# Keeping the split weights of two expert passes in device memory, and moving one wait of TensorE from layer 1 to layer 2

## The chip, the cores and the metric

The program runs on one core of a Trainium2 chip. The metric is the device time of one execution in microseconds (us), the median over several runs. A core has the matrix engine TensorE (PE in the profile), the vector engine VectorE (DVE), ScalarE (ACT), GpSimd (POOL) and SyncE (SP), which here issues most of the transfers; 16 DMA engines carry them.

## The reference, cut to what matters

Three parts follow each other: a windowed attention with block summaries, a dense mixture of 4 experts, and a mixture of 8 experts in which each token goes to one. The change is in the dense mixture. It takes the 1536 rows of x (two batches of 768 rows, 512 wide) through every expert e:

```python
p = domain_probs / (domain_probs.sum(-1, keepdims=True) + 1e-09)
out = np.zeros((N, D), dtype=np.float32)
for e in range(E):                      # E = 4, D = 512, F = 1024
    h = np.maximum(x @ w1[e], 0.0)      # layer 1
    out += p[:, e:e + 1] * (h @ w2[e])  # layer 2
```

The weights of an expert are the same for both batches.

## The kernel before

**Three matmuls for one.** TensorE gets each float32 operand as a high part (rounded by ScalarE's copy) and a low part (the rest, a subtraction on VectorE); a product is hi·hi + hi·lo + lo·hi.

**Passes.** Expert 0, and expert 3 of the second batch, run in a plain form, in groups of 384 rows. The five others are passes, `PASSES` = (batch 0, experts 1, 2, 3), (batch 1, experts 1, 2), numbered t = 0 to 4; `SWITCH` = 3 is the first pass of batch 1. A pass does layer 1 for a whole batch with seven block products in the place of eight (a Strassen-Winograd scheme, so each w1 is needed as seven blocks A12, S1, A11, A22, S2, S4, S3: three are quarters of w1, four are sums or differences of quarters, 256x512 each; x as its quarters and four sums T1 to T4). It is done in four turns of seven products (`factors`, six matmuls each by two halves of the inner axis: 168 matmuls), and then layer 2 in six tiles of 128 rows (`rows_out`, 144 matmuls, 24 a tile).

**Layer 1's weights.** SP loads the four quarters of w1 into `w_raw` (`load_blocks`, semaphores `block_sent`) when all products of the pass before are through (`product`). VectorE makes four sums in place (`block_sums`), ScalarE copies each of the seven blocks to `wb_hi` (`high_block`), and VectorE subtracts (`low_blocks`), which puts `wb_lo` over `w_raw` and raises `block_ok`. All this lies in time beside layer 2 of the pass before: `between(t, tt)` says what VectorE does after it has added tile tt of pass t to `acc` (`add_more`, line 1370). TensorE may begin tile m when `rows_added` is m-1, since two PSUM banks take turns. `load_second` brings w2 of the pass into places of `acc` and `v2_raw_end` when layer 2 of the pass before is through (`rows_done`).

**The switch of batches.** At t = 3 the x of batch 1 comes back from `x_aside`, its four sums T1 to T4 are made again (`first_sum` and the like, line 1290 on, and their split `high_sum` and `low_sum`, line 1320), and the finished rows of batch 0 are stored.

**Order of work.** It is written out by hand for each engine. SP's list of transfers is one queue in order: a wait in it holds all that stands behind.

Of the kernel before, what the change touches and what calls it, by code (L numbers as in the profile page):

```python
# [7 lines left out]
F32 = mybir.dt.float32  # L8
# [7 lines left out]
P = 128  # L16


def sparse_attention_moe_moe(nc, q, k, v, dprobs, w1, w2, w_skip, w_gate, v1, v2, out):
# [28 lines left out]
    G = 4  # L48
    GT = N // G
    GR = GT // P  # L50
# [21 lines left out]
    HALF_F = F // 2  # L72
# [39 lines left out]
    x1_rows = nc.dram_tensor("x1_rows", (N, D), F32).ap()  # L112
    route_list = nc.dram_tensor("route_list", (QT * COLS, 2), F32).ap()
    x_aside = nc.dram_tensor("x_aside", (2, P, KC, S), F32).ap()

    qh = q.rearrange("b h s d -> (b h) s d")
    kh = k.rearrange("b h s d -> (b h) s d")
# [2 lines left out]
    with ExitStack() as ctx:  # L120
# [3 lines left out]
        def sem(name):  # L124
            return ctx.enter_context(nc.semaphore(name))
# [193 lines left out]
        def block_part(parts, k):  # L319
            return parts[:, k, :, :].rearrange("p c f -> p (c f)")  # L320

        def x_block(d, t):

            return tuple(x[:, HALF_D * d:HALF_D * (d + 1), t * GT:(t + 1) * GT].bitcast(F32) for x in (xt_hi, xt_lo))
# [54 lines left out]
            sem("l1_done"), sem("h_hi_ok"), sem("h_ok"), sem("l2_done"), sem("acc_ok"))  # L379
        x_saved, x_back, acc_saved, acc_back = sem("x_saved"), sem("x_back"), sem("acc_saved"), sem("acc_back")  # L380
        block_sent = [sem(f"block_sent{k}") for k in range(4)]
        block_sum, block_hi_ok, block_ok = sem("block_sum"), sem("block_hi_ok"), sem("block_ok")
        t_step, t_sum, t_pool, t_hi_ok, t_ok = sem("t_step"), sem("t_sum"), sem("t_pool"), sem("t_hi_ok"), sem("t_ok")
        product, put_by, joined = sem("product"), sem("put_by"), sem("joined")
        hb_hi_ok, hb_ok = sem("hb_hi_ok"), sem("hb_ok")
        v2_sent = [sem(f"v2_sent{k}") for k in range(3)]
# [30 lines left out]
        def _(sp):  # L417
# [108 lines left out]
            def load_blocks(t):  # L526

                w = w1[PASSES[t][1]]
                for k, (to, row, col) in enumerate(((A12, 1, 0), (S4, 0, 1), (A22, 1, 1), (A11, 0, 0))):
                    sp.dma_start(w_raw[:, to, :, :], w[row * HALF_D * P:(row + 1) * HALF_D * P, col * HALF_F:(col + 1) * HALF_F].rearrange(  # L530
                        "(c p) f -> p c f", p=P)).then_inc(block_sent[k], 16)

            def load_second(t):

                b, e = PASSES[t]
                at = v2_at(b, 0)
                for k in range(2):
                    sp.dma_start(acc[:, at + 3 * k:at + 3 * k + 3, :], w2[e][3 * k * P:(3 * k + 3) * P, :].rearrange("(f p) d -> p f d", p=P)).then_inc(v2_sent[k], 16)
                sp.dma_start(v2_raw_end[:, :, :], w2[e][6 * P:8 * P, :].rearrange("(f p) d -> p f d", p=P)).then_inc(v2_sent[2], 16)
# [48 lines left out]
            sp.dma_start(late, acc[:, TPH:2 * TPH, :]).then_inc(acc_saved, 16)  # L588
            sp.wait_ge(acc_saved, 16)
            load_second(0)  # L590
            for t in range(1, len(PASSES)):
                sp.wait_ge(product, BLOCKS * FP * t)
                load_blocks(t)
                if t == SWITCH:
                    for j, x in enumerate((xt_hi, xt_lo)):
                        sp.dma_start(x[:, 0:KC, :].bitcast(F32), x_aside[j]).then_inc(x_back, 16)
                sp.wait_ge(rows_done, TPH * t)
                if t == SWITCH:
                    sp.dma_start(acc[:, TPH:2 * TPH, :], late).then_inc(acc_back, 16)
                    for g in range(HALVES):  # L600
                        keep(g)
                        send_out(g)
                    sp.wait_ge(x1_kept, 16 * HALVES)
                    sp.wait_ge(x1_out, 16 * HALVES)
                    sp.wait_ge(x1_tr, TPH)
                load_second(t)
            sp.wait_ge(product, BLOCKS * FP * len(PASSES))
            for c in range(PIECES):
                sp.dma_start(stage[:, c, :], w1_piece(w1[E1 - 1], c)).then_inc(w1_in[c], 16)
# [196 lines left out]
        def _(act):  # L806
# [137 lines left out]
            def high_blocks(t):  # L944

                for j in BLOCK_ORDER:
                    high_block(t, j)
                    if t in (0, SWITCH) and j in T_AFTER:
                        high_sum(PASSES[t][0], T_AFTER[j])

# [59 lines left out]
            high_blocks(0)  # L1010
            for t in range(len(PASSES)):
                factors(t)
                if t + 1 < len(PASSES):
                    high_blocks(t + 1)
                if t >= SWITCH:
                    route_exp(t - SWITCH)
# [80 lines left out]
        def _(dve):  # L1097
# [239 lines left out]
            def low_blocks(t, part):  # L1337
                for k in part:
                    j = BLOCK_ORDER[k]
                    dve.wait_ge(block_hi_ok, BLOCKS * t + k + 1)  # L1340
                    TT(block_part(wb_lo, j), block_in(j), block_part(wb_hi, j).bitcast(F32), ALU.subtract).then_inc(block_ok, 1)  # L1341
                    if t in (0, SWITCH) and j in T_AFTER:
                        low_sum(PASSES[t][0], T_AFTER[j])

            def low_second(t, k):
                f = ROW_ORDER[k]
# [203 lines left out]

            def between(t, tt):

                if t + 1 == SWITCH:
                    if tt == 0:
                        block_sums(t + 1, 0)
                        block_sums(t + 1, 1)
                    if tt == 1:
                        low_blocks(t + 1, range(1))
                    if tt == 2:
                        first_sum(1)  # L1560
                        second_sum(1)
                    if tt == 3:
                        fourth_sum(1)
                        third_sum(1)
                    if tt == 4:
                        low_blocks(t + 1, range(1, 4))
                    if tt == 5:
                        low_blocks(t + 1, range(4, BLOCKS))
                    return
                if t + 1 < len(PASSES):  # L1570
                    if tt == 0:
                        block_sums(t + 1, 0)
                        block_sums(t + 1, 1)
                    if tt == 1:
                        low_blocks(t + 1, range(3))
                    if tt == 2 and t < SWITCH:
                        low_blocks(t + 1, range(3, BLOCKS))
                    if tt == 4 and t >= SWITCH:
                        low_blocks(t + 1, range(3, BLOCKS))
                elif tt == 1:  # L1580
                    low_w1(1, lambda j: stage[:, j, :], [0, 1, 2])
                if t >= SWITCH:
                    if tt == 0:
                        choose(t - SWITCH)
                    if tt == 2:
                        places(t - SWITCH)
                    if tt == 3:
                        enter(t - SWITCH)
                    if tt == 4:
                        early_sum(t - SWITCH)  # L1590
# [165 lines left out]
        def _(pe):  # L1756
# [256 lines left out]
            def block(t, j, i, moving, bank, onto=False):  # L2013

                hi, lo = moving
                if i == 0:
                    pe.wait_ge(block_ok, BLOCKS * t + BLOCK_ORDER.index(j) + 1)
# [40 lines left out]
            def rows_out(t, fill):  # L2058

                b = PASSES[t][0]  # L2060
                for tt in range(TPH):
                    m = TPH * t + tt
                    if m >= 2:
                        pe.wait_ge(rows_added, m - 1)
                    for k, f in enumerate(ROW_ORDER):
                        if tt == 0:
                            pe.wait_ge(v2_ok, FC * t + k + 1)
                        if tt == 0 and k % 2 == 0:
                            pe.wait_ge(hb_ok, 4 * FP * t + 2 * k + 4)
# [13 lines left out]
            pe.wait_ge(o_lo, TASKS)  # L2083
            pe.wait_ge(pt_ready, 2 * TASKS)
            pe.wait_ge(h_ok, 2 + FC * G)
            pe.wait_ge(acc_ok, 2 + GR * G)
            for t in range(len(PASSES)):
                factors(t, route_fill if t == SWITCH else lambda k: None)

# [174 lines left out]
```

## Time and profile before

| | |
|---|---|
| median of 3 runs | 738.4 us (737.93 to 740.21) |
| profiled execution | 737.88 us, its span 736.1 us, so 1.8 us lie around the span |
| TensorE busy | 707.5 us, 96% |
| VectorE, ScalarE, GpSimd busy | 427.6, 291.6, 68.1 us |
| moved by DMA | 101.60 MB, mean 138 GB/s |
| the five passes | from 216.4 to about 538 us of the span |

The busy shares are means over stages with different limits. How a stage moves the end is read from the waits of the engine that is busy nearly all the time.

### The profile page before, as it was taken

The page shows a single profiled execution, that of the slowest core. Times are in us where ns is not written, and L with a number is a line of the kernel's source. Part 1 is how long each engine was busy: PE and PEld are TensorE (multiplying, and loading weights), DVE is VectorE, ACT ScalarE, POOL GpSimd, SP SyncE. Part 2 cuts the span into 40 slices and gives each one's busy share as a digit, 9 for nine tenths or more (in the row PEclk, how much of TensorE's full clock was granted, in tenths as well). Part 3 has the DMA queues.
Part 4 walks back from the last instruction along what each step waited for, and adds up shares of the span by engine and source line. Part 5 has one row for each costly group of instructions (what it writes and reads, how often), then busy time and mean ns, then how long its engine had stood idle before and what let it go on. Part 6 is the DMA issues. An engine that isn't in the chain of part 4 may idle for free.

```text
span 736.1 us, 12384 instructions
## 1 busy us (share of the span) xinstructions
PE 707.5 (96%) x4530; PEld 583.7 (79%) x4531; DVE 427.6 (58%) x1061; ACT 291.6 (40%) x651; POOL 68.1 (9%) x97
## 2 busy tenths in 40 slices
PE   5789999999989999999999999999999999999997
PEld 4578898888979889989988897898898985444444
DVE  4877674452976764782769469666542255544341
ACT  3655454351436614632624455056031202533430
POOL 2612000000000000000000000200100012332221
PEclk9999999999999999999999999999999999999999
DMA  9894732111523303213070723123224279599900
GB/s 200 215 219 94 145 68 63 42 37 62 225 76 124 115 1 116 74 41 115 1 285 9 280 84 115 24 91 115 86 86 172 87 287 356 204 396 396 386 8 21
DMA packets 88240, 101.60 MB, mean 138 GB/s; under 512 B 54617, under 2 KB 54893, under 8 KB 87281
## 3 DMA queue, kind: packets, MB, share of 16 engines
q1 hardware_dynamic: 85520, 96.14, 40.5%
q0 software_dynamic: 2656, 4.66, 2.0%
q8 instruction: 35, 0.57, 0.3%
q14 instruction: 29, 0.23, 0.1%
HBM read 88.32 MB, written 12.96 MB: 138 GB/s over the span
## 4 chain that ended last, share of the span: by engine, by line
PE 78%; DVE 12%; DMA 5%; issue 2%; SPq 1%; ACT 1%; POOL 0%; POOLq 0%; DVEq 0%; ACTq 0%
PE ps L1761 14%; PE ps L1763 14%; PE ps L1762 14%; PE ps L2023 6%; PE ps L2025 6%; PE ps L2024 6%; PE ps L2172 4%; PE ps L2144 4%; DMA sets<-in_moe_w 3%; DVE wb_lo L1341 2%; PE ps L1823 1%; PE ps L1795 1%; PE ps L1969 1%; PE ps L1809 1%; DVE xt_lo L1320 1%
## 5 line engine op out<-in xcount | busy, mean ns | idle before, releaser
L2023 PE MATMUL ps<-xt_hi,wb_hi 128*128 128x384 f32 x280 | 94.1, 336 | 4.8 <-DVE acc L1206 3.0
L2025 PE MATMUL ps<-xt_hi,wb_lo 128*128 128x384 f32 x280 | 93.6, 334 | 0.0
L2024 PE MATMUL ps<-xt_lo,wb_hi 128*128 128x384 f32 x280 | 93.6, 334 | 0.0
L954 ACT ACTIVATE h_raw<-ps 128x384 f32<-128x384 f32 x80 | 39.3, 491 | 90.8 <-PE ps L2025 88.9
L1762 PE MATMUL ps<-v_lo_acc,hb_hi 128*128 128x512 f32 x180 | 70.1, 390 | 0.0
L1761 PE MATMUL ps<-xt_hi,w_hi 128*128 128x384 f32 x184 | 64.2, 349 | 0.3 <-DVE h_lo L1197 0.3
L1355 DVE TENSOR_TENSOR h_raw<-ps,h_raw 128x384 f32<-128x384 f32 x80 | 41.4, 553 | 37.3 <-PE ps L2025 37.3
L1763 PE MATMUL ps<-xt_hi,w_lo 128*128 128x384 f32 x184 | 61.8, 336 | 0.0
L890 ACT ACTIVATE h_hi<-ps 128x384 fp32r<-128x384 f32 x48 | 23.6, 492 | 96.2 <-PE ps L1763 71.0
L1762 PE MATMUL ps<-xt_lo,w_hi 128*128 128x384 f32 x184 | 61.6, 335 | 0.0
L960 ACT ACTIVATE hb_hi<-h_raw 128x384 fp32r<-128x384 f32 x80 | 40.9, 526 | 45.3 <-DVE h_raw L1355 45.2
L1761 PE MATMUL ps<-w_hi,h_hi 128*128 128x512 f32 x144 | 58.1, 404 | 0.0
L2023 PEld LDWEIGHTS ps<-xt_hi,wb_hi 128*128 128x128 f32 x280 | 52.6, 188 | 5.6 <-issue 3.4
L1763 PE MATMUL ps<-w_hi,h_lo 128*128 128x512 f32 x144 | 56.4, 391 | 0.0
L1762 PE MATMUL ps<-w_lo,h_hi 128*128 128x512 f32 x144 | 56.2, 390 | 0.0
L2024 PEld LDWEIGHTS ps<-xt_lo,wb_hi 128*128 128x128 f32 x280 | 52.6, 188 | 0.2
L2144 PE MATMUL ps<-sets,acc 128*64 128x512 f32 x224 | 51.6, 599 | 1.1 <-DVE sets L1702 0.6
L2025 PEld LDWEIGHTS ps<-xt_hi,wb_lo 128*128 128x128 f32 x280 | 52.6, 188 | 0.0
L2172 PE MATMUL ps<-sets,acc 128*64 128x256 f32 x448 | 51.6, 382 | 0.7 <-ACT acc L1041 0.7
L1370 DVE SCALAR_TENSOR_TENSOR acc<-ps,dp,acc 128x512 f32<-128x512 f32 x30 | 22.5, 750 | 48.1 <-PE ps L1763 48.1
L1360 DVE SCALAR_TENSOR_TENSOR hb_lo<-h_raw,hb_hi 128x384 fp32r<-128x384 f32 x80 | 42.2, 555 | 12.0 <-ACT hb_hi L960 11.9
L1197 DVE SCALAR_TENSOR_TENSOR h_lo<-ps,h_hi 128x384 fp32r<-128x384 f32 x48 | 26.6, 555 | 37.3 <-ACT h_hi L890 37.2
(268 smaller groups left out, 1402.9 us busy)
## 6 DMA issues: line engine op xcount, KB each, us to landing
sets<-in_moe_w SPq DMA_DIRECT2D x72, 512.0 KB, 5.0
w_raw<-in_moe_w SPq DMA_DIRECT2D x20, 512.0 KB, 5.3
acc<-in_moe_w SPq DMA_DIRECT2D x10, 768.0 KB, 5.3
stage<-in_moe_w SPq DMA_DIRECT2D x8, 512.0 KB, 4.5
stage<-in_k SPq DMA_DIRECT2D x16, 192.0 KB, 4.8
acc<-in_v SPq DMA_DIRECT2D x4, 768.0 KB, 6.8
x_rows<-acc SPq DMA_DIRECT2D x4, 768.0 KB, 6.7
out_rows<-acc SPq DMA_DIRECT2D x4, 768.0 KB, 8.3
```

Of the source, the lines that this page charges most:

```text
L954: nc.scalar.activation(h_raw[:, f, half * GT:(half + 1) * GT], ps[:, bank, 0:GT], ACT.Copy).then_inc(put_by, 1)
L960: nc.scalar.activation(hb_hi[cols], h_raw[cols], ACT.Relu).then_inc(hb_hi_ok, 1)
L1355: TT(to, ps[:, bank, 0:GT], to, ALU.add).then_inc(joined, 1)
L1360: nc.vector.scalar_tensor_tensor(out=hb_lo[cols], in0=h_raw[cols], scalar=0.0, in1=hb_hi[cols].bitcast(F32), op0=ALU.max, op1=ALU.subtract ...
L1761: mm(dst, a_hi, b_hi, start=start, stop=False)
L1762: mm(dst, a_hi, b_lo, start=False, stop=False)
L1763: return mm(dst, a_lo, b_hi, start=False, stop=stop)
L2023: mm(to, wb_hi[w], hi(c), start=(c == 0 and not onto), stop=False, skip_group_check=onto)
L2024: mm(to, wb_hi[w], lo(c), start=False, stop=False, skip_group_check=onto)
L2025: last = mm(to, wb_lo[w], hi(c), start=False, stop=(c == HALF_D - 1), skip_group_check=onto)
L2144: last = mm(ps[j * QT:(j + 1) * QT, 0, 0:FQ], xt2[:, from_c:from_c + QT], wset[:, 0, at:at + FQ], start=(c == 0), stop=(c == KC - 1))
L2172: last = mm(ps[j * QT:(j + 1) * QT, bank, 0:DQ], ht2[:, at:at + QT], wset[:, 0, to:to + DQ], start=(f == 0), stop=(f == FC - 1))
```

## The change

- After pass 0's and pass 1's split blocks are made, SP stores `wb_hi` and `wb_lo` to a new tensor `w_aside` in device memory (`save_blocks`): two DMAs a pass, each 128 x 7168 floats, 3.67 MB, one run of 28,672 bytes a partition. They stand behind `load_second` of the same pass.
- `load_blocks` of passes 1 and 2 waits, beside `product`, for these stores (`blocks_saved`).
- Passes 3 and 4 use experts 1 and 2 again. Their blocks come back by 14 DMAs of 0.52 MB each (`blocks_again`), straight to `wb_hi` and `wb_lo`; there is no `load_blocks`, no sum, no high and no low part of blocks for them. TensorE waits for the DMAs (`block_back`, three semaphores: A12; S1 and A11; the four others).
- At t = 3 the load of x stands ahead of the blocks' load, and VectorE's sums and low parts of x are spread anew over the tiles.
- TensorE's wait for the last additions of the plain groups (`acc_ok`) moves from ahead of pass 0's layer 1 to its layer 2.

```diff
@@ -530,6 +537,18 @@
+            def save_blocks(t):
+
+                sp.wait_ge(block_ok, BLOCKS * (t + 1))
+                for j, x in enumerate((wb_hi, wb_lo)):
+                    sp.dma_start(w_aside[t, j], x[:, :, :, :].bitcast(F32)).then_inc(blocks_saved, 16)
+
+            def blocks_again(t):
+
+                for j in BLOCK_ORDER:
+                    for k, x in enumerate((wb_hi, wb_lo)):
+                        sp.dma_start(x[:, j, :, :].bitcast(F32), w_aside[t - SWITCH, k, :, j]).then_inc(block_back[back_part(j)], 16)
@@ -588,12 +607,17 @@
             load_second(0)
+            save_blocks(0)
             for t in range(1, len(PASSES)):
                 sp.wait_ge(product, BLOCKS * FP * t)
-                load_blocks(t)
                 if t == SWITCH:
                     for j, x in enumerate((xt_hi, xt_lo)):
                         sp.dma_start(x[:, 0:KC, :].bitcast(F32), x_aside[j]).then_inc(x_back, 16)
+                if t >= SWITCH:
+                    blocks_again(t)
+                else:
+                    sp.wait_ge(blocks_saved, 32 * min(t, KEPT))
+                    load_blocks(t)
                 sp.wait_ge(rows_done, TPH * t)
...
                 load_second(t)
+                if t < KEPT:
+                    save_blocks(t)
@@ -1550,34 +1577,28 @@
             def between(t, tt):
 
-                if t + 1 == SWITCH:
-                    if tt == 0:
-                        block_sums(t + 1, 0)
-                        block_sums(t + 1, 1)
-                    if tt == 1:
-                        low_blocks(t + 1, range(1))
...
+                if t + 1 == SWITCH:
+                    if tt == 1:
+                        first_sum(1)
+                    if tt == 2:
+                        second_sum(1)
+                        fourth_sum(1)
+                        low_sum(1, T1)
+                    if tt == 3:
+                        third_sum(1)
+                        low_sum(1, T4)
+                    if tt == 4:
+                        low_sum(1, T2)
+                        low_sum(1, T3)
@@ -2058,6 +2082,8 @@
             def rows_out(t, fill):
 
                 b = PASSES[t][0]
+                if t == 0:
+                    pe.wait_ge(acc_ok, 2 + GR * G)
@@ -2083,7 +2109,6 @@
             pe.wait_ge(h_ok, 2 + FC * G)
-            pe.wait_ge(acc_ok, 2 + GR * G)
```

SP's queue from the end of the plain groups to the blocks of pass 1, before (w_raw is where the quarters of w1 land, v2_raw_end and the acc places where w2 lands):

```order
L588 DMA x1_rows<-acc 128x6x512 [waits acc_ok]
L538 DMA acc<-in_moe_w2 128x3x512 [waits acc_saved]
L538 DMA acc<-in_moe_w2 128x3x512
L539 DMA v2_raw_end<-in_moe_w2 128x2x512
L530 DMA w_raw<-in_moe_w1 128x2x512 [waits product]
L530 DMA w_raw<-in_moe_w1 128x2x512 x3
```

The same place in the changed kernel:

```order
L607 DMA x1_rows<-acc 128x6x512 [waits acc_ok]
L557 DMA acc<-in_moe_w2 128x3x512 [waits acc_saved]
L557 DMA acc<-in_moe_w2 128x3x512
L558 DMA v2_raw_end<-in_moe_w2 128x2x512
L544 DMA w_aside<-wb_hi 128x7168 [waits block_ok]
L544 DMA w_aside<-wb_lo 128x7168
L537 DMA w_raw<-in_moe_w1 128x2x512 [waits blocks_saved,product]
L537 DMA w_raw<-in_moe_w1 128x2x512 x3
```

Two large stores now stand between, and the load of w1's quarters waits for them as well as for the products.

VectorE at the switch, its last work beside layer 2 of pass 2 and the first of pass 3, before (wb_lo are low parts of blocks, xt_lo those of x's sums, acc is a tile's addition, h_raw a joining of layer 1):

```order
L1370 SCALAR_TENSOR_TENSOR acc<-ps,dp,acc 128x512 [waits rows_done]
L1341 TENSOR_TENSOR wb_lo<-w_raw,wb_hi 128x1024 [waits block_hi_ok]
L1320 TENSOR_TENSOR xt_lo<-x_raw,xt_hi 128x768 [waits t_hi_ok]
L1341 TENSOR_TENSOR wb_lo<-w_raw,wb_hi 128x1024 [waits block_hi_ok] x2
L1320 TENSOR_TENSOR xt_lo<-x_raw,xt_hi 128x768 [waits t_hi_ok]
L1355 TENSOR_TENSOR h_raw<-ps,h_raw 128x384 [waits put_by,product]
```

The same place in the changed kernel:

```order
L1397 SCALAR_TENSOR_TENSOR acc<-ps,dp,acc 128x512 [waits rows_done]
L1347 TENSOR_TENSOR xt_lo<-x_raw,xt_hi 128x768 [waits t_hi_ok] x2
L1397 SCALAR_TENSOR_TENSOR acc<-ps,dp,acc 128x512 [waits rows_done]
L1382 TENSOR_TENSOR h_raw<-ps,h_raw 128x384 [waits put_by,product]
L1387 SCALAR_TENSOR_TENSOR hb_lo<-h_raw,hb_hi 128x384 [waits hb_hi_ok]
```

Nothing stands any more between the last tile's addition and the first joining of pass 3.

## Rows read from the trace of the kernel before

**Rows 1.** The page, busy time of the engines

```profile
PE 707.5 (96%) x4530; PEld 583.7 (79%) x4531; DVE 427.6 (58%) x1061; ACT 291.6 (40%) x651; POOL 68.1 (9%) x97
```

**Rows 2.** Windows: layer 1 of pass 0, and of pass 3 (stretch, length, busy times, clock, DMA)

```profile
213.60:245.80 32.20, 29.36 (x169) 29.39 (x170) 20.44 (x39) 16.87 (x35) 0.00 (x0) 1.00 0.32 115
402.40:443.00 40.60, 38.86 (x248) 38.21 (x248) 24.05 (x41) 20.11 (x42) 0.00 (x0) 1.00 0.50 170
```

**Rows 3.** Timeline before pass 0: start, length, engine, line, idle before and releaser

```profile
215.44 0.74 DVE L1206 TENSOR_SCALAR acc<-ps,dp 128x512 f32<-128x512 f32 x1
216.44 0.41 PE L2023 MATMUL ps<-xt_hi,wb_hi 128*128 128x384 f32 x1 [3.02 <-DVE acc L1206]
```

**Rows 4.** Timeline at the start of pass 3, VectorE and TensorE

```profile
405.43 2.36 DVE L1341 TENSOR_TENSOR wb_lo<-w_raw,wb_hi 128x1024 fp32r<-128x1024 f32 x2
408.57 0.56 DVE L1355 TENSOR_TENSOR h_raw<-ps,h_raw 128x384 f32<-128x384 f32 x1
...
407.11 0.34 PE L2025 MATMUL ps<-xt_hi,wb_lo 128*128 128x384 f32 x1
409.18 0.45 PE L2023 MATMUL ps<-xt_hi,wb_hi 128*128 128x384 f32 x1 [1.74 <-DVE h_raw L1355]
```

**Rows 5.** Instructions on tile w_raw: ns min/median/max of one

```profile
L935 ACT ACTIVATE wb_hi<-w_raw x35: 1041/1046/1064, 197.5 to 454.6; 128x1024 fp32r<-128x1024 f32 x35
L1341 DVE TENSOR_TENSOR wb_lo<-w_raw,wb_hi x35: 1214/1219/1225, 202.7 to 473.8; 128x1024 fp32r<-128x1024 f32 x35
```

**Rows 6.** ScalarE's first high part of w2 in pass 0; landing of DMAs on acc, 216 to 240

```profile
226.50 0.64 ACT L968 ACTIVATE v_hi_first<-acc 128x512 fp32r<-128x512 f32 x1
...
DMA to landing us min/median/max: 4.5/5.8/7.2
```

**Rows 7.** Timeline of SP's DMA issues

```profile
179.61 1.93 SPq L530 DMA_DIRECT2D w_raw<-in_moe_w  x4
...
222.00 1.37 SPq L538 DMA_DIRECT2D acc<-in_moe_w  x2
223.42 0.49 SPq L539 DMA_DIRECT2D v_raw_end<-in_moe_w  x1
245.83 1.91 SPq L530 DMA_DIRECT2D w_raw<-in_moe_w  x4
...
278.59 0.90 SPq L538 DMA_DIRECT2D acc<-in_moe_w  x2
...
307.74 1.91 SPq L530 DMA_DIRECT2D w_raw<-in_moe_w  x4
...
369.65 1.90 SPq L530 DMA_DIRECT2D w_raw<-in_moe_w  x4
```

**Rows 8.** Stores of x aside: issue time; size and us to landing; then w2's last part

```profile
L544 SPq DMA_DIRECT2D x_aside<-xt_lo x1: 438/438/438, 182.1 to 182.1; - x1
...
x_aside<-xt_lo SPq DMA_DIRECT2D x1, 1536.0 KB, 15.1
...
v_raw_end<-in_moe_w SPq DMA_DIRECT2D x1, 512.0 KB, 7.5
```

**Rows 9.** Windows: DMA rate (last number, GB/s) in stores of x and of acc

```profile
190.00:192.00 2.00, 2.00 (x13) 2.00 (x12) 1.68 (x4) 0.49 (x1) 0.00 (x0) 1.00 0.95 406
192.00:194.00 2.00, 2.00 (x14) 2.00 (x13) 1.97 (x3) 0.49 (x1) 0.00 (x0) 1.00 1.06 444
218.00:220.00 2.00, 2.00 (x14) 2.00 (x13) 0.10 (x1) 0.74 (x2) 0.00 (x0) 1.00 1.02 378
```

**Rows 10.** Timeline beside layer 2 of pass 0: first block sum, second addition, fourth tile

```profile
253.02 1.22 DVE L1327 TENSOR_TENSOR w_raw<-w_raw 128x1024 f32<-128x1024 f32 x1 [0.93 <-DMA w_raw<-in_moe_w]
257.92 0.74 DVE L1370 SCALAR_TENSOR_TENSOR acc<-ps,dp,acc 128x512 f32<-128x512 f32 x1
...
262.04 0.39 PE L1761 MATMUL ps<-v_hi_first,hb_hi 128*128 128x512 f32 x1
```

**Rows 11.** Window in the routed stage: DMA rate of loads of 4 KB runs

```profile
650.00:660.00 10.00, 10.00 (x74) 5.13 (x72) 4.80 (x11) 4.15 (x5) 4.19 (x4) 1.00 1.04 394
```

More of the change, by code:

```diff
@@ L114, in sparse_attention_moe_moe @@
     x_aside = nc.dram_tensor("x_aside", (2, P, KC, S), F32).ap()
+    KEPT = len(PASSES) - SWITCH
+    w_aside = nc.dram_tensor("w_aside", (KEPT, 2, P, BLOCKS, HALF_D, HALF_F), F32).ap()
     qh = q.rearrange("b h s d -> (b h) s d")
@@ L320, in block_part, with back_part @@
             return parts[:, k, :, :].rearrange("p c f -> p (c f)")
+        def back_part(j):
+            return 0 if j == A12 else 1 if j in (S1, A11) else 2
         def x_block(d, t):
@@ L381, in sparse_attention_moe_moe @@
         block_sent = [sem(f"block_sent{k}") for k in range(4)]
+        blocks_saved = sem("blocks_saved")
+        block_back = [sem(f"block_back{k}") for k in range(3)]
         block_sum, block_hi_ok, block_ok = sem("block_sum"), sem("block_hi_ok"), sem("block_ok")
-        t_step, t_sum, t_pool, t_hi_ok, t_ok = sem("t_step"), sem("t_sum"), sem("t_pool"), sem("t_hi_ok"), sem("t_ok")
+        t_step, t_sum, t_hi_ok, t_ok = sem("t_step"), sem("t_sum"), sem("t_hi_ok"), sem("t_ok")
         product, put_by, joined = sem("product"), sem("put_by"), sem("joined")
@@ L946, in high_blocks @@
                 for j in BLOCK_ORDER:
-                    high_block(t, j)
+                    if t < SWITCH:
+                        high_block(t, j)
                     if t in (0, SWITCH) and j in T_AFTER:
@@ L1012, in _ @@
                 factors(t)
-                if t + 1 < len(PASSES):
+                if t + 1 <= SWITCH:
                     high_blocks(t + 1)
@@ L1341, in low_blocks @@
                     TT(block_part(wb_lo, j), block_in(j), block_part(wb_hi, j).bitcast(F32), ALU.subtract).then_inc(block_ok, 1)
-                    if t in (0, SWITCH) and j in T_AFTER:
-                        low_sum(PASSES[t][0], T_AFTER[j])
+                    if t == 0 and j in T_AFTER:
+                        low_sum(0, T_AFTER[j])
             def low_second(t, k):
@@ L1551, in between @@
             def between(t, tt):
-                if t + 1 == SWITCH:
-                    if tt == 0:
-                        block_sums(t + 1, 0)
-                        block_sums(t + 1, 1)
-                    if tt == 1:
-                        low_blocks(t + 1, range(1))
[L1559 to L1570, printed above, removed]
+                if t + 1 < SWITCH:
                     if tt == 0:
@@ L1575, in between @@
                         low_blocks(t + 1, range(3))
-                    if tt == 2 and t < SWITCH:
+                    if tt == 2:
                         low_blocks(t + 1, range(3, BLOCKS))
-                    if tt == 4 and t >= SWITCH:
-                        low_blocks(t + 1, range(3, BLOCKS))
-                elif tt == 1:
+                if t + 1 == SWITCH:
+                    if tt == 1:
+                        first_sum(1)
+                    if tt == 2:
+                        second_sum(1)
[7 more added lines that the diff above has]
+                        low_sum(1, T3)
+                if t + 1 == len(PASSES) and tt == 1:
                     low_w1(1, lambda j: stage[:, j, :], [0, 1, 2])
@@ L2016, in block @@
                 if i == 0:
-                    pe.wait_ge(block_ok, BLOCKS * t + BLOCK_ORDER.index(j) + 1)
+                    if t < SWITCH:
+                        pe.wait_ge(block_ok, BLOCKS * t + BLOCK_ORDER.index(j) + 1)
+                    else:
+                        pe.wait_ge(block_back[back_part(j)], 32 * (1, 2, 4)[back_part(j)] * (t - SWITCH + 1))
                     if t in (0, SWITCH) and j in T_AFTER:
```

## The prediction

> **What bounds the kernel now.** The page first: TensorE is busy 96% of the span, VectorE and ScalarE 58% and 40% [rows 1]. So what these two are spared is worth nothing by itself; only the gaps of TensorE count, and I looked for them with the windows, one for each half of a pass, and the waits of PE in each. In all five passes TensorE loses about 5 us, at two places that the change touches. In the window of pass 0's layer 1 it is busy 29.36 of 32.20 us, in that of pass 3's layer 1 38.86 of 40.60 [rows 2]. The others are full, but for 0.3 us at the first tile of pass 3's layer 2.
>
> The first gap is 3.02 us: pass 0's first product waits for VectorE's last plain addition, which ends at 216.1, behind block work [rows 3]. The second is 1.74 us: TensorE's fifth product of pass 3 waits for the joining that stands on VectorE behind four low parts of blocks and x's sums; these end at 408.57, where the joining begins [rows 4]. Both show VectorE late at a boundary. What follows has to be read from SP's queue, since that is where the change puts its new work.
>
> **Part 1, block work left out in passes 3 and 4.** VectorE is spared 2 x (4 sums + 7 low parts) at 1.22 us, 26.8 us, and ScalarE 2 x 7 x 1.05 = 14.7 us [rows 5]. Beside layer 2 of pass 3 they hid behind full TensorE: nothing. At the switch the 1.74 us go: in the new order nothing stands between the last addition and the joining, and x's sums are spread over the four tiles before. Nothing else of that boundary is near: ScalarE waited on VectorE there too. I take -1.7 us.
>
> **Part 2, the blocks' way back.** At the switch 3.15 MB of x and 7.34 MB of blocks (14 x 0.52) are loaded, issued from 369.65 [rows 7] by 16 issues of some 0.48 us. At 394 GB/s, the rate of loads in 4 KB runs [rows 11], 10.5 MB take 26.6 us; with 5.4 us for start and end (worked out below) all have landed at 401.7. Pass 3 begins at 402.3, the fourth product, the first that wants the last group, some 4 us later. The cover is thin for the last blocks (4 to 5 us) and wide for A12. Before pass 4 there are 7.34 MB, 24 us in a stretch of 33: hidden. If the rate fell to 330 GB/s, 5.2 us would be added at the switch and the cover would just be gone. Cost taken: 0.
>
> **Part 3, TensorE's wait moved.** Pass 0's layer 1 can start 3.0 us earlier; its blocks are ready (the last low part and the sum T4's are wanted six products later). But SP's order is unchanged: w2's first part is issued at 222.00 and lands 4.5 us later, at 226.5, the moment when ScalarE starts its high part [rows 6, 7]. Moved 3 us ahead, ScalarE stands in this wait, and behind it in its list are the high part of the hidden rows and the `put` copies that free TensorE's banks; w2's second part (landing 7.2 us after 222.4 [rows 6]) is met the same way at 229.6. Following that chain, VectorE's joinings come at 230.7 where they were at 230.9. So TensorE keeps about 0.8 us of the 3.0 (from 0.5 up to all of it, if ScalarE's order gives more slack than I see).
>
> **Part 4, the stores.** Pass 0's two stores, 7.34 MB, stand behind w2's three loads (2.10 MB, issued from 222.00, last landing 223.42 + 7.5 = 230.9 [rows 7, 8]) and ahead of w1's quarters for pass 1, which were issued at 245.83 when layer 1 was through. When do they land? The nearest rows are x's stores: runs of 12 KB a partition, 406 to 444 GB/s [rows 9], I take 428. From 179.61, the first issue, to the last landing at 182.1 + 15.1 = 197.2 [rows 7, 8] a load of 2.10 MB and stores of 3.15 MB take 17.6 us; 5.24 MB at 428 are 12.2, so start, change from loads to stores, and last landing cost 5.4. Here: 9.44 MB / 428 = 22.1, + 5.4, from 222.0: 249.5. Worked from the other end: stores flow from some 229.5, 17.1 us, + 1.5 for the change + 2.2 for the last landing: 250.3. I take 250.0, with 247.5 (no loss but the landing) and 253.0 (378 GB/s, acc's store in 2 KB runs [rows 9]) as bounds.
>
> So w1's quarters are issued 4.2 us later than before. Who waits: VectorE's sums stand in its list between the first and the second tile's additions, and start when the quarters land, at 253.02; the second addition ends at 257.92 + 0.7, 12.8 us behind the issue (a later pass shows 12.2), and TensorE begins the fourth tile at 262.04, which needs that addition [rows 7, 10]. The issue may come at 262.0 - 12.5 = 249.5 and cost nothing against before; with 250.0 TensorE is 0.5 us behind the old kernel there, whatever it had gained at the start. The gain of part 3 is thus eaten by the store: **+0.5 us** for parts 3 and 4 together, from -0.8 to +3.5.
>
> Pass 1's stores: w2 is issued at 278.59, layer 1 ends at 307.74 [rows 7], so 29.1 us and the same 3.7 us of slack; 9.44 MB want 27.5 to 29. Hidden, and still so at 378 GB/s (31).
>
> **What the skill says of the rate.** The Trainium skill, "DMA: Bandwidth & Descriptors", Specifications, gives about 358 GB/s as HBM's limit for a core; its page "HBM Reference" (Specifications) limits this to both cores of a pair at work and has about 425 for one alone. The trace agrees with the second: 406 to 444. By the first the stores would take 20.5 us in place of 17.1, which would add 3.4 us.
>
> **Sum.** -1.74 + 0.5 = -1.2 us (part 2 adds 0). Against the profiled execution's own time, 737.88: **736.7 us**. This execution is 0.5 us below the median shown (738.4); a median of the new kernel may lie as much above my figure. What comes behind pass 4 is tied to TensorE's steps and moves with it.
>
> **Rivals.**
> - *Both gaps are given back.* If the stores land by 248, the issue costs nothing and part 3's gain stays: -1.7 - 0.8 to -1.7 - 1.5, so 734.7 to 735.4. If ScalarE had slack too and the stores landed by 246.3, all 4.8 us: 733.1. For it: runs of 28 KB, the longest in the program, may go faster than those of 12. Against: 7.34 MB in 17 us is already the best rate seen.
> - *The stores are slow* (the other side). Loads and stores mixed run slower in this trace, and no store of this length is in it. One mechanism: the store of pass 0 holds w1's quarters, VectorE stands in the wait for them, the second addition is late, and TensorE stops at the fourth tile of layer 2. Each us of landing beyond 249.5 is one us; it outweighs the 1.7 from a landing at 251.2, and gives over 2.2 us from 253.4, which is 375 GB/s by the same sum. At 330 GB/s: landing 255.1, +5.6 - 1.7, and pass 1 adds 0.5: 742. At 230 GB/s: 14.8 us more in pass 0, 10 in pass 1, 762.
> - *The stores run a sixth slower than x's*, at some steady ceiling: 17.1 us become 20.5, the landing 253.4, +3.9 - 1.7 = +2.2, 740.1. For it, acc's stores at 378 GB/s [rows 9]; against it, x's at 406 to 444. This is what the Trainium skill's first limit above would do.
> - *The blocks come back late at pass 3*, TensorE waiting on `block_back`: below 330 GB/s only. It would come along with slow stores.
>
> **How the numbers follow.** About 0.3%, 2.2 us, is what a measurement of this kernel tells from no change. Forecast, landing from 249 to 253, net -2.2 to +2.0: 0.52. Gaps given back: 0.26, of which all of it 0.04. Stores slow: 0.14. A sixth slower: 0.08, half of it over +2.2. Faster then is 0.28, same 0.53, slower 0.19. The range goes from 734.6 (the first rival's near end) to 741.5 (stores near 335 GB/s); about 0.1 lies beyond each end.
>
> **What would show it.** Pass 0's first product at about 213.4, without the wait for `acc`. ScalarE's first high part of w2 still at 226.5, now after a wait for a DMA. Two stores with a last landing near 250, and w1's quarters issued then, not at the end of layer 1. VectorE waiting some 4 us for `w_raw` beside layer 2 of pass 0, and TensorE a new wait of about 1.3 us (0.8 + 0.5) on `acc` at its fourth tile. No such wait in pass 1. No wait at pass 3's fifth product, and none on blocks. I am wrong if stores run below 375 or above 450 GB/s, if TensorE keeps more of the first 3 us, or if transfers of this size slow the engines' own instructions.

## The result, and the profile of the changed kernel

The changed kernel takes 737.5 us (median of 20 runs, 735.54 to 739.88), the kernel before 739.41 in 20 runs beside it (736.84 to 742.14). The ratio of the runs taken side by side is 0.997, 95% interval 0.9958 to 0.9983: 2.2 us less, from 1.3 to 3.1 (the two medians are 1.9 apart). The profiled execution took 737.65 us, its span 735.9.

The page first: span, busy times, one group of layer 2 and the DMAs of the change (KB each, us to landing).

```profile
span 735.9 us, 12370 instructions
...
PE 708.9 (96%) x4530; PEld 585.1 (80%) x4531; DVE 402.9 (55%) x1039; ACT 277.6 (38%) x637; POOL 66.3 (9%) x97
...
L1782 PE MATMUL ps<-v_hi_first,hb_hi 128*128 128x512 f32 x120 | 47.2, 393 | 1.5 <-DVE acc L1397 1.5
...
w_aside<-wb_hi SPq DMA_DIRECT2D x2, 3584.0 KB, 16.6
w_aside<-wb_lo SPq DMA_DIRECT2D x2, 3584.0 KB, 24.8
wb_hi<-w_aside SPq DMA_DIRECT2D x14, 512.0 KB, 11.9
```

Against [rows 1] VectorE has 22 instructions and 24.7 us less, ScalarE 14 and 14.0 us less. TensorE has as many matmuls as before, and a wait of 1.5 us at layer 2 that it did not have.

The waits of TensorE from the start of pass 0 to the start of pass 1's first sums (213 to 265 us): for what, us in total, times, longest.

```profile
PE ps L1782 <- DVE acc L1397: 1.5, 1, 1.5
PE ps L2047 <- ACT h_raw L981: 1.4, 1, 1.4
PE ps L2047 <- DVE h_raw L1382: 0.4, 1, 0.4
```

In place of one wait of 3.02 us [rows 3] there are three, 3.2 us together (ps is the bank in PSUM that a matmul writes, h_raw the joined sums of layer 1). The timeline shows where they stand: the last plain matmul, the first product right behind it, two products at layer 1, and the fourth tile of layer 2.

```profile
213.99 0.39 PE L1784 MATMUL ps<-w_hi,h_lo 128*128 128x512 f32 x1
214.22 0.33 PE L2047 MATMUL ps<-xt_hi,wb_hi 128*128 128x384 f32 x1
...
229.30 0.45 PE L2047 MATMUL ps<-xt_hi,wb_hi 128*128 128x384 f32 x1 [1.37 <-ACT h_raw L981]
...
232.02 0.45 PE L2047 MATMUL ps<-xt_hi,wb_hi 128*128 128x384 f32 x1 [0.35 <-DVE h_raw L1382]
...
263.72 0.50 PE L1782 MATMUL ps<-v_hi_first,hb_hi 128*128 128x512 f32 x1 [1.50 <-DVE acc L1397]
```

ScalarE and VectorE show what is late behind each. ScalarE stands 3.16 us in the wait for w2's first part, and once more for its second, with the copies that free TensorE's banks behind it; VectorE waits 5.90 us for w1's quarters, and the second addition starts at 262.92.

```profile
227.45 0.63 ACT L995 ACTIVATE v_hi_first<-acc 128x512 fp32r<-128x512 f32 x1 [3.16 <-DMA acc<-in_moe_w]
...
230.14 0.63 ACT L995 ACTIVATE v_hi_next<-acc 128x512 fp32r<-128x512 f32 x1 [0.90 <-DMA acc<-in_moe_w]
...
258.00 1.23 DVE L1354 TENSOR_TENSOR w_raw<-w_raw 128x1024 f32<-128x1024 f32 x1 [5.90 <-DMA w_raw<-in_moe_w]
...
262.92 0.75 DVE L1397 SCALAR_TENSOR_TENSOR acc<-ps,dp,acc 128x512 f32<-128x512 f32 x1
```

SP's issues give the landings: w1's quarters go out as soon as the last store has landed, 24.7 us behind its issue at 225.33 (the page's 24.8 is the median of pass 0's and pass 1's).

```profile
222.97 0.92 SPq L557 DMA_DIRECT2D acc<-in_moe_w  x2
223.93 0.49 SPq L558 DMA_DIRECT2D v_raw_end<-in_moe_w  x1
224.46 0.82 SPq L544 DMA_DIRECT2D w_aside<-wb_hi  x1
225.33 0.46 SPq L544 DMA_DIRECT2D w_aside<-wb_lo  x1
250.15 1.92 SPq L537 DMA_DIRECT2D w_raw<-in_moe_w  x4
...
280.38 0.90 SPq L557 DMA_DIRECT2D acc<-in_moe_w  x2
```

Windows over the stores, over the end of the blocks' way back, and over layer 1 of pass 3 (the last two numbers are the DMA share and GB/s, the one before them the clock):

```profile
235.00:237.00 2.00, 2.00 (x14) 2.00 (x13) 1.16 (x2) 1.45 (x4) 0.00 (x0) 1.00 1.06 459
...
243.00:245.00 2.00, 2.00 (x14) 2.00 (x13) 1.19 (x3) 1.24 (x3) 0.00 (x0) 1.00 0.94 401
...
396.00:398.00 2.00, 2.00 (x10) 1.65 (x10) 1.77 (x2) 0.85 (x1) 0.00 (x0) 1.00 1.04 416
398.00:400.00 2.00, 2.00 (x11) 1.64 (x10) 1.25 (x2) 0.00 (x0) 0.00 (x0) 1.00 0.31 125
...
404.19:441.31 37.12, 37.12 (x241) 37.08 (x241) 17.18 (x32) 19.44 (x40) 0.00 (x0) 1.00 0.52 185
```

The last block's issue stands at 383.88 and its landing 16.8 us behind, at 400.7, 3.5 us before pass 3, and in its layer 1 TensorE is full: the 1.74 us of [rows 4] are gone.

**Two stretches to compare by.** The whole times of two kernels differ by little more than their scatter, and in the profiles below pass 0 begins anywhere from 212 to 216 us, whatever the kernel; that is settled before 180 us, where the kernels are alike (section on the hardware). So I compare two stretches. **A** runs from the start of TensorE's last plain matmul to SP's issue of w2 for pass 1, that is over the seam and all of pass 0. **B** runs from the end of pass 2 (SP's `acc<-x_rows`) to the end of pass 3's layer 1 (SP's next issue for weights). By the single profile of before, A went from 65.56 (213.03 to 278.59) to 66.39 (213.99 to 280.38), +0.8; B from 39.12 (402.41 to 441.53) to 37.12, -2.0. Together -1.2, what was forecast, where the timed runs say -2.2. Between A and B, and from B to the end, the two are equal within 0.1 us; up to A's start the changed profile is 0.96 longer, which is the scatter just named. That the one profile gives just what was forecast is in part luck; the runs below show why the timed runs say more.

### The profile page after: what moved, and what is told of

Its sections match the earlier page's. It is cut to its first block, busy times and chain, and to the rows that moved or that the text cites. A ratio compares the mean times of both kernels' runs of the same rounds, so it can differ in the third digit from the quotient of the medians.

```text
span 735.9 us, 12370 instructions
## 1 busy us (share of the span) xinstructions
PE 708.9 (96%) x4530; PEld 585.1 (80%) x4531; DVE 402.9 (55%) x1039; ACT 277.6 (38%) x637; POOL 66.3 (9%) x97
## 4 chain that ended last, share of the span: by engine, by line
PE 76%; DVE 10%; DMA 9%; issue 2%; SPq 1%; ACT 1%; POOL 0%; DVEq 0%; POOLq 0%
PE ps L1782 14%; PE ps L1784 14%; PE ps L1783 14%; PE ps L2047 5%; PE ps L2049 5%; PE ps L2048 5%; PE ps L2197 4%; PE ps L2169 4%; DMA w_aside<-wb_lo 3%; DMA sets<-in_moe_w 3%; PE ps L1844 2%; PE ps L1816 2%; PE ps L1990 1%; PE ps L1830 1%; DVE wb_lo L1368 1%
## 5 line engine op out<-in xcount | busy, mean ns | idle before, releaser
L1782 PE MATMUL ps<-xt_hi,w_hi 128*128 128x384 f32 x184 | 64.2, 349 | 0.3 <-DVE h_lo L1224 0.3
L1782 PE MATMUL ps<-v_hi_first,hb_hi 128*128 128x512 f32 x120 | 47.2, 393 | 1.5 <-DVE acc L1397 1.5
## 6 DMA issues: line engine op xcount, KB each, us to landing
w_aside<-wb_lo SPq DMA_DIRECT2D x2, 3584.0 KB, 24.8
```

The lines of the kernel that those rows point to most:

```text
L1782: mm(dst, a_hi, b_hi, start=start, stop=False)
```

## The experiments

All of them, with what the profile of each gave. "Clock" is the granted TensorE clock between 217 and 223 us. The ratio of each run is to executions of the kernel before taken beside it, whose medians were 739.41 for the changed kernel, 739.93 for no_store0, wait_back, wait_only and store_twice, 739.98 for low_first, low_first_early, after_again and wait_back_again, and 740.35 for the last four. So two runs of different groups are compared by their ratios, not by their medians.

| kernel | median us | ratio to before (interval) | A | B | clock |
|---|---|---|---|---|---|
| before | 739.41 | 1 | 65.56 | 39.12 | 1.00 |
| changed | 737.5 | 0.997 (0.9958 to 0.9983) | 66.39 | 37.12 | 1.00 |
| no_store0 | (718.9) | not comparable | 64.34 | 37.11 | 1.00 |
| wait_back | 738.17 | 0.9983 (0.9968 to 0.9998) | 67.15 | 37.11 | 0.72 |
| wait_only | 737.6 | 0.9976 (0.9951 to 1.0001) | 64.37 | 39.12 | 1.00 |
| store_twice | 754.56 | 1.0202 (1.0179 to 1.0224) | 84.73 | 37.11 | 1.00 |
| low_first | 735.6 | 0.9937 (0.9914 to 0.9959) | 65.18 | 37.11 | 1.00 |
| low_first_early | 734.16 | 0.9906 (0.9875 to 0.9937) | 62.87 | 37.11 | 1.00 |
| after_again | 737.64 | 0.9966 (0.9944 to 0.9989) | 65.78 | 37.11 | 1.00 |
| wait_back_again | 738.55 | 0.9965 (0.9946 to 0.9985) | 68.23 | 37.12 | 0.52 |
| before_again | 739.63 | 0.9995 (0.9965 to 1.0024) | 66.92 | 39.12 | 0.78 |
| before_again_2 | 739.8 | 0.9992 (0.9964 to 1.002) | 67.12 | 39.12 | 0.72 |
| busy_switch | 738.53 | 0.9972 (0.9951 to 0.9993) | 65.35 | 38.35 | 1.00 |
| best_again | 733.38 | 0.9906 (0.9875 to 0.9937) | 62.82 | 37.11 | 1.00 |

**1. No store in pass 0** (no_store0). The changed kernel without pass 0's two stores. Pass 3 then takes the blocks of expert 2 in the place of expert 1's, so the routed stage sorts its tokens otherwise and takes another time: the whole time can't be compared, A can.

```diff
             load_second(0)
-            save_blocks(0)
...
-                if t < KEPT:
+                if t == 1:
                     save_blocks(t)
```

> The changed kernel without pass 0's stores; passes 3 and 4 both take pass 1's blocks, so pass 3 computes with another expert's w1 and the loads stay as many. Yardstick, in each profile: from TensorE's last plain matmul to the issue of pass 1's w2 (before 65.6 us, changed 66.4). Theory (the store holds w1's quarters, and that alone makes the wait at the fourth tile): quarters issued at the end of layer 1, no wait at the fourth tile, yardstick 64.7; the switch as in the changed kernel; whole time 1.7 us under the changed kernel's, some 2.9 us or 0.4% under before. Rival (pass 0 is late for w2's landing alone): the yardstick stays at 66.4.

A is 64.34 where the theory had 64.7. SP issues w1's quarters at 244.61, at the end of layer 1, and there is no wait at the fourth tile. ScalarE's wait is still there: TensorE has one wait of 1.7 us for `h_raw`, but the one of 0.4 for the joining is gone. So the stores cost 66.39 - 64.34 = 2.0 us of A in the first profile of the changed kernel; by the mean of its three (65.84, below) it is 1.5.

**2. The wait set back** (wait_back). The changed kernel with TensorE's wait for `acc_ok` again ahead of layer 1.

```diff
             def rows_out(t, fill):
-                if t == 0:
-                    pe.wait_ge(acc_ok, 2 + GR * G)
...
+            pe.wait_ge(acc_ok, 2 + GR * G)
```

> The changed kernel with TensorE's wait for the plain additions back ahead of layer 1. Theory (the store's landing sets the fourth tile, whatever layer 1 gained): yardstick stays at 66.4 us (within 0.2), the 3 us wait returns at the start, the waits for put and joining in layer 1 go, the wait at the fourth tile shrinks from 1.5 to about 0.5. Rival (the moved wait is worth what layer 1 shows, 1.1 us): yardstick 67.5.

**3. The wait moved alone** (wait_only). The kernel before, with that one line moved and nothing else.

> The kernel before with nothing but TensorE's wait moved to layer 2. Theory (w2's first landing on ScalarE eats most of the 3 us): ScalarE waits about 3 us for w2's first part, TensorE about 1.4 and 0.4 us in layer 1, yardstick 64.5 in place of 65.6; the 1.7 us at pass 3 stay; whole time 1.0 us (0.14%) under before. Rival (the whole of the 3 us is kept where no store is in the way): yardstick 62.4.

Wait_only gives A = 64.37. It is 1.2 us shorter than the 65.56 of before, and equal to no_store0: with no stores, the moved wait keeps 1.2 us of its 3.0. The rival of a TensorE that keeps all of it, 62.4, is dead. (Both A here come from profiles whose clock stayed up.) B is 39.12, with the old wait in it, so the moved wait has no part in what the switch gave. ScalarE waits here as in the changed kernel.

```profile
226.30 0.63 ACT L968 ACTIVATE v_hi_first<-acc 128x512 fp32r<-128x512 f32 x1 [3.44 <-DMA acc<-in_moe_w]
...
228.16 0.44 PE L2023 MATMUL ps<-xt_hi,wb_hi 128*128 128x384 f32 x1 [1.66 <-ACT h_raw L954]
```

Wait_back came out longer than I could account for. It has one wait of 3.0 us in all of pass 0, as before has, w1's quarters go out at 250.80, and yet A is 67.15, not 65.6. The window behind the pause shows why: the clock.

```profile
217.00:223.00 6.00, 6.00 (x27) 6.00 (x26) 0.67 (x2) 1.65 (x4) 0.00 (x0) 0.72 0.72 264
```

27 matmuls where the changed kernel does 37 in the same 6 us. (1 - 0.72) x 6 = 1.7 us are lost, and 67.15 - 1.7 = 65.5 would be before's A. With the wait set back there is also no wait at the fourth tile, so there the stores cost nothing. This was in no theory of mine, and led to runs 7 to 10.

**4. Pass 0's stores twice** (store_twice), the second time to another tensor that nothing reads. The load of w1's quarters waits for all four stores.

```diff
+                if t == 0:
+                    for j, x in enumerate((wb_hi, wb_lo)):
+                        sp.dma_start(w_twice[j], x[:, :, :, :].bitcast(F32)).then_inc(blocks_saved, 16)
```

> The changed kernel with pass 0's two stores done a second time to another tensor, and the quarters of w1 waiting for all four; nothing else. Theory (beyond its slack each us of landing is one us of the whole): 7.34 MB more at 440 GB/s are 16.7 us, quarters issued at 266.9 in place of 250.2, TensorE's wait at the fourth tile 18.2 us in place of 1.5, yardstick 83.1, whole time about 754. Rival (VectorE's queue has slack that hides part): less than 12 us more.

754.56 us (two executions), 17 more than the changed kernel. SP issues w1's quarters at 265.40, and this row of the waits shows the whole price in one place:

```profile
PE ps L1786 <- DVE acc L1401: 17.5, 1, 17.5
```

The path is the one that the prediction named: store, quarters of w1, VectorE's sums, second addition, fourth tile. Once past the slack, a microsecond of landing is a microsecond of time. A is 84.73, some 1.6 us over what I expected, and the windows behind the pause show the rest: the clock is half while TensorE waits, and not yet full in the 6 us behind. TensorE goes on at 278.49 and its matmuls are slow until 282.05, which costs half of 3.6 us, 1.8.

```profile
268.00:274.00 6.00, 0.00 (x0) 0.00 (x0) 1.24 (x2) 1.06 (x1) 0.00 (x0) 0.50 0.78 277
...
280.00:286.00 6.00, 6.00 (x24) 4.83 (x23) 6.00 (x7) 0.00 (x0) 0.00 (x0) 0.83 0.01 3
```

**5. The low parts' store first** (low_first). w1's quarters land in the place of `wb_lo` alone. So the low parts are stored first and SP waits only for them; ScalarE, which writes `wb_hi`, waits for the other store.

```diff
-                for j, x in enumerate((wb_hi, wb_lo)):
-                    sp.dma_start(w_aside[t, j], x[:, :, :, :].bitcast(F32)).then_inc(blocks_saved, 16)
+                for j, x, saved in ((1, wb_lo, low_saved), (0, wb_hi, high_saved)):
+                    sp.dma_start(w_aside[t, j], x[:, :, :, :].bitcast(F32)).then_inc(saved, 16)
...
-                    sp.wait_ge(blocks_saved, 32 * min(t, KEPT))
+                    sp.wait_ge(low_saved, 16 * min(t, KEPT))
...
             def high_blocks(t):
+                if 0 < t < SWITCH:
+                    act.wait_ge(high_saved, 16 * min(t, KEPT))
```

> The changed kernel with two gates in place of one: the store of wb_lo goes first, w1's quarters wait for it alone (they land on wb_lo), and ScalarE's high parts of the next blocks wait for the store of wb_hi. Theory: wb_lo's store has landed before layer 1 ends, so the quarters are issued there, some 4.5 us earlier than in the changed kernel (31.5 us after the last plain matmul, not 36.2), they travel behind the rest of wb_hi's store but land in time, the wait at the fourth tile is gone, yardstick 64.4 us in place of 66.4; whole time 2.0 us under the changed kernel, 0.4 to 0.45% under before. Rival (the bytes in the queue count, not the gate): quarters land as late as before behind wb_hi, fourth tile still waits 1 us or more.

735.6 us. The quarters are issued at 245.92, the end of layer 1, and the wait at the fourth tile is gone. A is 65.18 where I expected 64.4. The 0.8 us are in layer 1: TensorE waits 1.7 and 0.6 us for `h_raw`, where no_store0 and wait_only have the first of these waits alone.

**6. The same, with w2 earlier** (low_first_early). What holds w2 is the store of `acc`, which needs the last plain addition. Three low parts of blocks stood between the last two of these additions on VectorE; the third now stands behind the last.

```diff
             low_blocks(0, range(2, 4))
             add_rows(c, 0, c, 1, True)
-            low_blocks(0, range(4, BLOCKS))
+            low_blocks(0, range(4, 6))
             add_rows(c, 0, c, 2, True)
+            low_blocks(0, range(6, BLOCKS))
```

> As low_first, and VectorE's last plain addition stands ahead of the seventh block's low part, 1.9 us earlier, so that acc is stored and w2 loaded 1.9 us earlier. Theory (layer 1 of pass 0 loses its 1.4 to 1.7 and 0.4 us to w2's landing): TensorE's waits in layer 1 gone or under 0.3 us, yardstick 62.5 to 62.8; whole time 3.5 us under the changed kernel, about 0.6 to 0.65% under before. Rival (the late block part is now what layer 1 waits for): a wait of TensorE on t_ok or block_ok in its first turn, yardstick 64 or more.

734.16 us, and A = 62.87. `acc`'s store goes out 1.2 us behind the last plain matmul's start (216.25), not 3.2, and w2 with it; of TensorE's waits in A one of 0.3 us is left. Of the 3.0 us that the moved wait was to give, 65.56 - 62.87 = 2.7 are had once w2 comes earlier too: its issue stands 7.0 us behind the last plain matmul's start, in low_first 9.3. By its ratio it beats the kernel before and the changed one.

**7 and 8. The changed kernel and the one with the wait set back, once more** (after_again, wait_back_again).

> The changed kernel once more, for the spread of what lies ahead of pass 0. Theory: the stretch up to the last plain matmul scatters by about 1 us between executions of any kernel (213.0 before, 214.0 changed), the yardstick repeats at 66.4 within 0.4, the stretch from there to the end repeats within 0.3.

> The kernel wait_back once more: its first profile had the store of acc land 7.3 us after issue in place of 5.8 to 6.2, which delayed w2 and the stores by as much. Theory (the store's landing sets the fourth tile): with a landing at 5.8 to 6.2 us the yardstick is 65.9 to 66.4. Rival (the moved wait is worth 1.1 us): 67.2 again.

After_again: 737.64 us, ratio as the first time; A = 65.78, with waits of 1.7, 0.6 and 0.4 us. Its fourth tile waits 0.4 where the first profile shows 1.50: VectorE's sums begin 6.9 us behind the issue of w1's quarters (248.33 to 255.22), in the first profile 7.85 (250.15 to 258.00). Wait_back_again has A = 68.23 and the clock at 0.52 behind the pause. Neither the theory's nor the rival's length came out, since both left the clock out. The whole times can't tell the wait set back from the changed kernel: its ratios are 0.9983 and 0.9965, those of the changed kernel 0.997 and 0.9966, and the intervals overlap. In the group that has both, the medians are 738.55 and 737.64.

**9 and 10. The kernel before, twice more** (before_again, before_again_2). Nothing is changed; the question is its clock.

> The kernel before once more, nothing changed, timed like the others. Question: does the granted clock fall in the 6 us behind TensorE's pause of 3.0 us ahead of pass 0, as it did in both profiles of the wait set back, or not, as in the first profile of the kernel before? Theory of the clock: it falls in this one too; the stretch from the last plain matmul's start to pass 1's issue of w2 is 67 to 68.5 us. Rival: before's clock stays, and the stretch is 65.6 again; then the fall belongs to something in the changed kernel. The whole time is the same as the kernel's other runs, 739.4, ratio 1.000.

> A third profile of the kernel before, as the second: does the clock fall behind the pause of 3.0 us? Theory of the clock: in most profiles, stretch 67 to 68.5; where it doesn't fall, 65.6. Rival: never, 65.6 in all.

Both have the same wait of 3.02 us as [rows 3], and in both the clock falls behind it: 0.78 and 0.72, where the first profile has 1.00. The window, and matmuls from the slow stretch of before_again:

```profile
217.00:223.00 6.00, 6.00 (x28) 6.00 (x29) 0.81 (x2) 1.80 (x4) 0.00 (x0) 0.78 0.72 264
```

```profile
216.77 0.66 PE L2023 MATMUL ps<-xt_hi,wb_hi 128*128 128x384 f32 x1 [3.02 <-DVE acc L1206]
...
218.19 0.52 PE L2024 MATMUL ps<-xt_lo,wb_hi 128*128 128x384 f32 x1
218.51 0.52 PE L2025 MATMUL ps<-xt_hi,wb_lo 128*128 128x384 f32 x1
```

The same stretch of the changed kernel:

```profile
218.06 0.34 PE L2048 MATMUL ps<-xt_lo,wb_hi 128*128 128x384 f32 x1
218.23 0.33 PE L2049 MATMUL ps<-xt_hi,wb_lo 128*128 128x384 f32 x1
```

The starts are 0.32 us apart in the one and 0.17 in the other: TensorE runs at 1.2 and at 2.4 GHz. A becomes 66.92 and 67.12, against 65.56 in the profile that I predicted from.

**11. Work back at the switch** (busy_switch). The changed kernel, with x's sum T3 and its low part behind the last addition again.

```diff
                     if tt == 3:
-                        third_sum(1)
                         low_sum(1, T4)
                     if tt == 4:
                         low_sum(1, T2)
+                    if tt == 5:
+                        third_sum(1)
                         low_sum(1, T3)
```

> The changed kernel, but x's sum T3 (three additions) and its low part moved back behind VectorE's last addition at the switch, some 3 us of work ahead of the first joining of pass 3; T4's and T2's low parts stand a tile earlier. Theory: TensorE's 1.74 us at the fifth product came from what VectorE does between the last addition and the joining, so a wait of about 1 us comes back there, and the stretch from SP's issue of the blocks' way back being through (404.19 in the changed kernel) to layer 1's end (441.31) grows from 37.1 to 38.1 or 38.4. Whole time +1.0 to +1.3 on the changed kernel's 737.5. Rival: the gap went because of what stands on the DMA queues and ScalarE; no wait, the stretch stays 37.1.

The wait is back where it was, at the fifth product, and B grows from 37.12 to 38.35:

```profile
408.31 0.44 PE L2048 MATMUL ps<-xt_hi,wb_hi 128*128 128x384 f32 x1 [0.97 <-DVE h_raw L1382]
```

So the gap of [rows 4] came from VectorE's work between the last addition and the joining, and taking that work away is what removed it. A wait shown as 0.97 costs 1.23, as the one shown as 1.74 cost 2.0: 0.26 us on top of each. The whole time shows none of it: 738.53, ratio 0.9972, where the changed kernel has 0.997; its median was 1.0 above the changed kernel's, beside a before that was 0.9 above its own.

**12. The best version once more** (best_again).

> The version with the low parts' store first and the stores' and w2's order early, timed once more. It has no pause over 1 us between the plain groups and pass 1. Theory: 734.2 again, ratio 0.991 to 0.994; stretch 62.5 to 63; no fall of the clock behind the start of pass 0. Rival: the first result was chance, ratio that of the changed kernel, 0.997.

733.38 us, A = 62.82. The ratio and its interval are the same for both takes; the plain quotients of the medians are 0.9921 and 0.9906. Its interval (0.9875 to 0.9937) and that of the changed kernel beside before (0.9958 to 0.9983) do not touch.

## Why the prediction was right, point by point

The forecast, 736.7 us and -1.2 against the profiled execution, has the measured 737.5 in its range. The change comes out at the edge of what the text called no change: -2.2 us, where 2.2 was the bound. That the figure of 736.7 lies within 0.8 us of the median is in part luck: it starts from an execution of 737.88, 1.5 us under the median of before's 20 runs, and its gain is 1.0 short. Its terms:

- **Part 1, block work left out: -1.7, measured -2.0.** Right in cause (run 11) and place. 0.26 us were missing, since a pause costs TensorE more than the idle time shown.
- **Part 2, the way back: 0, measured 0.** I had all blocks landed 32.0 us behind the first issue of the switch (369.65 to 401.7); it was 29.3 (371.43 to 400.7), at 405 to 425 GB/s for most of the way where I took 394, and TensorE waits for none.
- **Part 3, the moved wait: 0.8 of the 3.0 us kept, measured 1.2** (runs 1 and 3). The mechanism is the predicted one: ScalarE stands in w2's wait with the copies that free TensorE's banks behind it. Run 6 shows it from the other side: with w2 2 us earlier relative to TensorE, 2.7 of the 3.0 are had.
- **Part 4, the stores.** w1's quarters were to be issued at 250.0, which is 37.0 us behind the last plain matmul's start; measured 36.2, 36.5 and 36.4 in three profiles. While the stores have the queue alone, the rate is 459 GB/s at its best, over the 428 taken, but 424, 401 and 373 in the 6 us from 241. The wait at the fourth tile was forecast as 1.3 us; it is 1.50, 0.4 and none in the three, by how soon the quarters land: the second addition ends 13.5, 12.6 and 12.1 us behind their issue, where I took 12.5. I had not expected the other wait that comes with the stores, 0.2 to 0.7 us at a joining in layer 1; it is in all seven profiles with pass 0's stores and the moved wait, and in neither of those without the stores (1 and 3). Pass 1's stores are hidden, as predicted: no wait there.
- **Parts 3 and 4 together: +0.5; measured +0.8 against the profile I had, and -0.7 against the mean of three** (changed, after_again and busy_switch, whose pass 0 is the same: 65.84; before: 66.53). This is where the forecast was short. I took the A of one profile of before, and in that one the clock had stayed up behind the 3.0 us pause. In the two others it fell, and cost 1.4 and 1.6 us. The changed kernel has no pause over 1.7 us there, and its clock stayed up in all its profiles. So the moved wait also spares what the clock took: -0.7 - 2.0 = -2.7, inside the measured 1.3 to 3.1, where -1.2 lies just outside. At full clock the two parts come to 65.84 - 65.56 = +0.3, close to the +0.5 forecast: beside the stores, what the moved wait gains is the clock.
- **The timed runs say the same of the clock.** Each has the mean granted clock of its execution. It is 0.9929 on average over the 95 timed with the kernel before in three groups, 0.9956 over the 32 of the changed kernel. Over a span of 736 us the difference is worth 2.0 us (an estimate), and the mean times, 740.4 and 737.4, differ by 3.0; what is left, -1.0, is near the -1.2 that was forecast without the clock. In the group of 739.98 the means are 0.9936 for before, 0.9939 for the wait set back, 0.9957 for the changed kernel and 0.9964 for low_first. The group of 739.93 is less clear: 0.9947 with the wait set back, 0.9950 in wait_only.

The rivals: "both gaps given back" was half true (of the first gap the moved wait keeps 1.2 us, and the stores spend it, run 1: 1.5 to 2.0 us). "The stores are slow" is dead: the last landing is 36.2 us behind the last plain matmul, not later than the 37.0 taken, though its path is real (run 4). So is "a sixth slower". One sum in the two doesn't hold: the landing at 253.4 is given for 375 GB/s in the first and for the sixth slower rate, 358, in the second; by 17.1 + 3.4 us for 7.34 MB it is 358. "The blocks come late" is dead too. By the page of the Trainium skill "DMA: Bandwidth & Descriptors" (Specifications, some 358 GB/s) the stores would have cost 3.4 us more, by the prediction's estimate; the trace, with windows of up to 459, does not agree with it, and is nearer to the 425 that "HBM Reference" (Specifications) has for one core alone.

## What to carry to other kernels

A wait taken from the busiest engine comes back at whichever load comes next: before moving it, move the load behind it by as much (run 6 kept 2.7 of 3.0 us, run 3 kept 1.2). When a buffer must be stored before it is refilled, store first the part that is refilled first, and wait for that part alone (run 5). And take a stretch that stands behind a pause of TensorE from several profiles, since one may show the clock up and the next down.

## What the runs showed of the hardware

- **The clock behind a pause.** In five profiles TensorE pauses 3.0 us ahead of pass 0, and in the 6 us behind it the granted clock is 1.00, 0.78, 0.72, 0.72 and 0.52. In the nine profiles without that pause it is 1.00 each time, and it stays 1.00 behind the waits of 1.4 to 1.7 us in layer 1 too. The loss is (1 - clock) x 6 us: 0, 1.3, 1.7, 1.7, 2.9, and A above 65.6 by 0, 1.3, 1.5, 1.6, 2.6. Behind the 17.5 us of run 4 it falls too. The Trainium skill, "TensorE: Matmul & The Clock Gate", Part 1, has 1.2 GHz for an idle array and 2.4 for a busy one, and says that the point of the change at a kernel's start varies from run to run; the traces show the same two levels, and a fall in four of five profiles. What decides it in an execution stays open.
- **A pause costs more than the wait shown.** In B it was 0.26 us more, for waits of 1.74 and 0.97. Add as much to every wait in A and count from before's 65.56, and A comes out within 0.2 us in the eight other profiles whose clock stayed up all through it: 66.3 for the 66.39 of the changed kernel with its three waits, 64.2 for the 64.37 of wait_only with one of 1.66, 62.8 for the 62.87 of low_first_early with one of 0.26. So one wait broken into three costs some 0.5 us more than their sum shows.
- **The start scatters.** In the first 48 us the clock falls, in twelve of the fourteen profiles and not at the same place, to 0.50 to 0.72 in the lowest 6 us. A begins anywhere from 211.83 to 216.02, at 213.99 and 211.83 in two profiles of the changed kernel. The fall alone doesn't set this: the two profiles without one begin A at 213.18 and 213.15. From 180 us on nothing differs: from w1's load at 178 to 183 us to the last plain matmul it is 33.4 us in all fourteen.
- **One store, two lengths.** `acc`'s store of 1.5 MB takes 5.8 us or 7.3 from issue to landing in two profiles of the same kernel (before_again_2 and before_again), with the same transfers around it. Where something waits for it, that can be 1.5 us of scatter with no cause that I could see; in these two it didn't show, since A is 67.12 with the short one and 66.92 with the long.
